# All denominators added by DMA, longer lags, and the result copied out of PSUM by VectorE

## The reference

```python
w = exp(weight_gen - max(weight_gen))          # over the 7 taps
w = w / (sum(w) + 1e-9)
x = sum_k w[b, s, h, k] * x_pad[b, s + k, h]   # 4 x 4096 tokens, 192 wide, 8 heads

h = x @ w_in                                   # 16384 x 192 @ 192 x 2048
P = a[0] + a[1] * h + a[2] * h**2 + a[3] * h**3
Q = 1.0 + abs(b[0]) * abs(h) + abs(b[1]) * h**2
out = (P / (Q + 1e-6)) @ w_out                 # 2048 x 192
```

## Time and profile before

| | |
|---|---|
| median of 3 runs | 1492.36 us (1492.22 to 1493.45) |
| profiled execution | 1492.54 us |
| its span | 1490.7 us |
| busy: PE / PEld | 1311.9 (88%) / 1175.2 (79%) us |
| busy: DVE | 1401.8 us (94%) |
| busy: ACT | 1185.8 us (80%) |
| busy: POOL | 1366.0 us (92%) |
| DMA, queue of GpSimd / of SyncE | 50.34 MB, 16.6% / 51.36 MB, 10.2% of 16 engines |
| granted TensorE clock, mean | 0.992 |

### The profile page before, as it was taken

The page is one execution under the profiler, slowest core; times in us unless marked ns, Lnnn a source line. Parts: engine busy times, 40 slices in busy tenths (PEclk is TensorE's granted clock), DMA queues, the critical chain, the costliest instruction groups (busy, mean ns, idle before and its releaser), DMA issues.

```text
span 1490.7 us, 19206 instructions
## 1 busy us (share of the span) xinstructions
PE 1311.9 (88%) x6912; PEld 1175.2 (79%) x6912; DVE 1401.8 (94%) x904; ACT 1185.8 (80%) x966; POOL 1366.0 (92%) x704
## 2 busy tenths in 40 slices
PE   0399999999999999999999999999999999998998
PEld 0278888888888888888888888888888888888897
DVE  3998999999999999999999999999999999999986
ACT  1287888888788888778788888788878888878896
POOL 1889999999999999999999999999999999999632
PEclk9899999999999999999999999999999999999999
DMA  3422322322331322331321332231232232232112
GB/s 95 124 43 65 83 69 61 82 51 66 82 80 50 82 56 61 82 82 51 79 66 51 82 82 61 69 82 43 74 82 72 58 82 53 61 79 53 29 45 64
DMA packets 26270, 101.87 MB, mean 68 GB/s; under 512 B 2968, under 2 KB 9236, under 8 KB 26256
## 3 DMA queue, kind: packets, MB, share of 16 engines
q0 software_dynamic: 9216, 50.34, 16.6%
q1 hardware_dynamic: 16752, 51.36, 10.2%
q10 hardware_dynamic: 288, 0.00, 0.0%
HBM read 38.78 MB, written 12.58 MB: 34 GB/s over the span
## 4 chain that ended last, share of the span: by engine, by line
issue 39%; POOL 31%; DMA 13%; ACT 7%; PE 5%; SPq 2%; DVE 2%; POOLq 1%; ACTq 0%
POOL prod L322 18%; DMA den<-beta 12%; POOL beta L352 6%; ACT den L451 3%; POOL conv L322 3%; PE hps L679 3%; PE ops L689 3%; ACT den L475 2%; POOL conv L326 2%; SPq L240 1%; ACT xt_hi L414 1%; POOL taps L391 1%; POOL taps L377 1%; POOL den L359 1%; DMA num<-in_moe_w_in 1%
## 5 line engine op out<-in xcount | busy, mean ns | idle before, releaser
L689 PE MATMUL ops<-wo,gate 128*128 128x192 f32 x4096 | 700.3, 327 | 49.2 <-DVE gate L604 49.2
L689 PEld LDWEIGHTS ops<-wo,gate 128*128 128x128 f32 x4096 | 673.2, 190 | 77.8 <-DVE gate L604 62.6
L326 POOL TENSOR_TENSOR conv<-conv,prod 128x768 f32<-128x768 f32 (+2 forms) x192 | 556.1, 2896 | 15.0
L604 DVE SCALAR_TENSOR_TENSOR gate<-num,coef,den 128x1536 f32<-128x1536 f32 (+1 forms) x192 | 445.7, 2321 | 4.1 <-issue 3.1
L451 ACT ACTIVATE den<-den,one_eps 128x1536 f32<-128x1536 f32 (+1 forms) x192 | 276.1, 1438 | 199.9 <-DMA den<-beta 199.0
L322 POOL TENSOR_TENSOR prod<-xwin,taps 128x768 f32<-128x768 f32 (+2 forms) x192 | 380.6, 1982 | 3.4
L623 DVE SCALAR_TENSOR_TENSOR num<-num,coef,hps 128x1536 f32<-128x1536 f32 (+1 forms) x192 | 314.3, 1637 | 6.8
L620 DVE TENSOR_TENSOR num<-num,hps 128x1536 f32<-128x1536 f32 (+1 forms) x192 | 300.4, 1565 | 13.9 <-ACT num L478 13.8
L478 ACT ACTIVATE num<-hps,coef 128x1536 f32<-128x1536 f32 (+1 forms) x192 | 285.4, 1486 | 0.0
L454 ACT ACTIVATE den<-den 128x1536 f32<-128x1536 f32 (+1 forms) x192 | 258.6, 1347 | 5.1
L352 POOL TENSOR_SCALAR beta<-den,absb 128x1536 f32<-128x1536 f32 (+1 forms) x128 | 233.5, 1824 | 30.9 <-ACT den L475 16.5
(11 more groups left out here) (53 smaller groups left out, 886.8 us busy)
## 6 DMA issues: line engine op xcount, KB each, us to landing
den<-beta POOLq DMA_DIRECT2D x64, 768.0 KB, 5.6
xwin<-in_x SPq DMA_DIRECT2D x30, 960.0 KB
out<-out_sb SPq DMA_DIRECT2D x32, 384.0 KB, 2.4
taps_raw<-in_weight_gen SPq DMA_DIRECT2D x32, 112.0 KB, 2.2
wo<-in_moe_w_out SPq DMA_DIRECT2D x1, 1536.0 KB, 13.5
num<-in_moe_w_in SPq DMA_DIRECT2D x2, 512.0 KB, 6.8
num<-in_moe_w_in SPq DMA_DIRECT2D x4, 256.0 KB, 7.7
xwin<-in_x SPq DMA_DIRECT2D x1, 768.0 KB
```

The lines of the kernel that those rows point to most:

```text
L326: pool.tensor_tensor(conv[parity][:, cols], conv[parity][:, cols], prod[k % 2][:, cols], ALU.add).then_inc(conv_steps, 1)
L604: dve.scalar_tensor_tensor(slot(gate, g), slot(num, g), coef[:, 0:1], slot(den, g), ALU.add, ALU.mult).then_inc(gate_ready, 1)
L689: last = pe.matmul(ops[:, j // 2, (j % 2) * D:(j % 2 + 1) * D], gate[:, g % GATE_RING, n * COLS + j * P:n * COLS + (j + 1) * P], wo[:, c, ...
```

## The change

All six groups are `DMA_GROUPS`, none is a `POOL_GROUP`. So ScalarE makes the scaled |h| and the square in every group, GpSimd only issues the six DMAs, and L352, L359 and L628 are gone. The lags are 2, 3 and 4 groups instead of 1, 2 and 3; `num` and `den` have four places for groups instead of three, `beta` three instead of two. For their memory the three scratch arrays of VectorE's first two convolutions share that of `gate`. The copy out of `ops` is a VectorE instruction in place of a ScalarE one, and with the longer lag it stands in g3's slot, and TensorE's wait for it in g4's. The three small instructions that make the root for the square stand earlier on VectorE, since g0 needs it.

```diff
-INVERT_LAG = 1
-GATE_LAG = 2
-LAG = 3
-RING = 3
+INVERT_LAG = 2
+GATE_LAG = 3
+LAG = 4
+RING = 4
 GATE_RING = 3
-POOL_GROUPS = (4,)
-DMA_GROUPS = (2, 5)
+BETA_RING = 3
+POOL_GROUPS = ()
+DMA_GROUPS = tuple(range(GROUPS))
...
-        beta = sb("beta", [P, 2, GW])
+        beta = sb("beta", [P, BETA_RING, GW])
         gate = sb("gate", [P, GATE_RING, GW])
+        dprod = [gate[:, n, 0:ROW] for n in range(3)]
...
@@ scalar: evacuate, and its call between the two activations of invert
-            def evacuate(s, parity, stored_needed):
-
-                act.wait_ge(gate_used, GROUPS * (s + 1))
-                if stored_needed:
-                    act.wait_ge(out_stored[parity], after_dmas(s - 2, parity))
-                act.activation(out_sb[parity][:, :].rearrange("p (c w) -> p c w", c=2),
-                               ops[:, :, 0:ROW // 2], ACT.Copy).then_inc(out_ready, 1)
...
-                            if q == EVACUATE_AT and not first:
-                                evacuate(t - 1, 1 - odd, stored_needed=not second)
...
@@ vector
+            def evacuate(s, parity, stored_needed):
+
+                dve.wait_ge(gate_used, GROUPS * (s + 1))
+                if stored_needed:
+                    dve.wait_ge(out_stored[parity], after_dmas(s - 2, parity))
+                dve.tensor_copy(out_sb[parity][:, :].rearrange("p (c w) -> p c w", c=2),
+                                ops[:, :, 0:ROW // 2]).then_inc(out_ready, 1)
...
                         dve.tensor_tensor(slot(den, g), slot(den, g), slot(beta, g), ALU.mult).then_inc(q_by_dve, 1)
+                    if q == EVACUATE_AT and not first:
+                        evacuate(t - 1, 1 - odd, stored_needed=not second)
```

More of the change, by code:

```diff
@@ L100, in conv_rational_ffn @@
         prod = [sb(f"prod{n}", [P, ROW]) for n in range(2)]
-        dprod = [sb(f"dprod{n}", [P, ROW]) for n in range(3)]
         conv = [sb(f"conv{n}", [P, ROW]) for n in range(2)]
@@ L346, in group @@
                     return
-                if not first or q >= 2:
-                    wait_q(pool, t if q >= 2 else t - 1, (q - 2) % GROUPS)
+                if not first or q >= BETA_RING:
+                    wait_q(pool, t if q >= BETA_RING else t - 1, (q - BETA_RING) % GROUPS)
                 pool.wait_ge(abs_ready, GROUPS * t + q + 1)
@@ L454, in invert, with tile @@
                 act.activation(slot(den, g), slot(den, g), ACT.Exp, scale=-1.0).then_inc(inv_q_ready, 1)
-            def tile(t, odd, first=False, second=False, xt_ahead=True, taps_ahead=True):
+            def tile(t, odd, first=False, xt_ahead=True, taps_ahead=True):
                 for q in range(GROUPS):
@@ L470, in tile @@
                         act.activation(slot(den, g), h_of(q), ACT.Abs, scale=absb[:, 0:1]).then_inc(abs_ready, 1)
-                        if not first or q >= 2:
-                            wait_q(act, t if q >= 2 else t - 1, (q - 2) % GROUPS)
+                        if not first or q >= BETA_RING:
+                            wait_q(act, t if q >= BETA_RING else t - 1, (q - BETA_RING) % GROUPS)
                         act.activation(slot(beta, g), h_of(q), ACT.Square, scale=root[:, 2:3]).then_inc(square_ready, 1)
@@ L492, in _ @@
             tile(0, 0, first=True)
-            tile(1, 1, second=True)
-            with act.Fori(2, TILES - 4, 2) as t:
-                tile(t, 0)
-                tile(t + 1, 1)
-            for t in range(TILES - 4, TILES):
+            with act.Fori(1, TILES - 3, 2) as t:
+                tile(t, 1)
+                tile(t + 1, 0)
+            for t in range(TILES - 3, TILES):
                 tile(t, t % 2, xt_ahead=t + 1 < TILES, taps_ahead=t + 3 < TILES)
@@ L500, in _ @@
                 invert(GROUPS * (TILES - 1) + q, TILES - 1, place((TILES - 1) % 2, q))
-            evacuate(TILES - 1, (TILES - 1) % 2, True)
         @block.vector
@@ L580, in _ @@
             pre_conv(0)
+            dve.wait_ge(root_guess, 1)
+            dve.reciprocal(root[:, 1:2], root[:, 0:1]).then_inc(root_inverse, 1)
+            dve.wait_ge(root_inverse, 1)
+            dve.scalar_tensor_tensor(root[:, 2:3], root[:, 1:2], absb[:, 1:2], root[:, 0:1], ALU.mult,
+                                     ALU.add).then_inc(root_twice, 1)
+            dve.wait_ge(root_twice, 1)
+            dve.tensor_scalar(root[:, 2:3], root[:, 2:3], 0.5, None, ALU.mult).then_inc(root_ready, 1)
             wi_lo_half(0)
@@ L605, in gate_of, with tile @@
                                          ALU.add, ALU.mult).then_inc(gate_ready, 1)
-            def tile(t, odd, first=False, xt_ahead=True, taps_ahead=True):
+            def tile(t, odd, first=False, second=False, xt_ahead=True, taps_ahead=True):
                 for q in range(GROUPS):
@@ L642, in _ @@
             tile(0, 0, first=True)
-            with dve.Fori(1, TILES - 3, 2) as t:
-                tile(t, 1)
-                tile(t + 1, 0)
-            for t in range(TILES - 3, TILES):
+            tile(1, 1, second=True)
+            with dve.Fori(2, TILES - 4, 2) as t:
+                tile(t, 0)
+                tile(t + 1, 1)
+            for t in range(TILES - 4, TILES):
                 tile(t, t % 2, xt_ahead=t + 1 < TILES, taps_ahead=t + 3 < TILES)
@@ L649, in _ @@
                 gate_of(GROUPS * (TILES - 1) + q, place((TILES - 1) % 2, q), True)
+            evacuate(TILES - 1, (TILES - 1) % 2, True)
         @block.tensor
```

7 lines of the change are left out of this document (removed).

## The result

| | before | after |
|---|---|---|
| median (range) | 1492.9 us (1492.22 to 1493.83) | 1601.21 us (1600.13 to 1602.62) |
| span of the profiled execution | 1490.7 us | 1598.3 us |
| tile in the settled stretch | 44.34 us | 47.78 us |
| granted TensorE clock, mean | 0.992 | 0.93 |

What follows compares the result with a forecast made beforehand. VectorE and GpSimd were taken to bound the old kernel; in the new one, 30 cycles through the late copy (1340.1 us) plus start and end gave 1511 us, and clock falls + 20: 1531 us, range 1493 to 1585.

Steps and rivals of the forecast that it cites:

- What bounded the kernel before: Settled stretch of the old kernel: VectorE and GpSimd together set the pace, at 44.34 us per tile.
- DMAs at nothing: Six DMAs per tile cost no time: landing plus a GpSimd step below 10 us, against some 14 us of cover.
- Rival (c): A DMA late, or VectorE held up by GpSimd at g3: 1540, up to 1590 with a falling clock; chance 0.08.
- ScalarE's slots, 41.05 us: ScalarE's own work over the six groups of a tile, summed to 41.05 us: the tile if nothing else came last.
- The path to the copy: From ScalarE's |h| of g3 through square, linear step and VectorE's num steps to the copy: 8.04 us, copy 0.94.
- The ring: Cycle ScalarE, VectorE's num steps, copy, TensorE's second product, back to ScalarE: 44.7 us per tile.
- rival (d): Copy ready early enough, so ScalarE's 41.05 us set the pace: 1401 us; chance 0.11 including its half, 1489.
- The end of TensorE's gap to ScalarE's |h| of g5: From TensorE's second product of g0, after waiting for the copy, to ScalarE's next three-chunk |h|: 7.68 us.
- at the edge: TensorE's new gap before the second product of g0, 4.1 us, is nearly the 4.30 us that cost the clock.
- eight of thirty: TensorE's clock falls behind the gap in eight of thirty tiles: + 20 us on 1511.
- rival (b): TensorE's clock falls behind the gap in nearly every tile: 1560 to 1590 us; chance 0.10.
- the price of a fall: Time TensorE's matmuls behind the gap lose when the clock halves: 2.5 us per tile.

## Why the prediction was wrong, step by step

- **What bounded the kernel before: held, with one reading that was too short.** VectorE and GpSimd set its pace: less of their work (copy ahead, all groups by DMA) gives 41.0 us per tile. But the 122.1 us of ScalarE for DMAs in the earlier trace rows went for another reason than the lag of two, as the runs with short lags show.
- **DMAs at nothing: right.** Three times as many, landing in 5.6 us in the median (4.4 for two chunks; 6.5 at the most from 500 to 1300 us), and no wait for one. Rival (c) did not occur.
- **ScalarE's slots, 41.05 us: right**, 41.02 where they bind. The square of two chunks, which had no row, took 1.00 (taken: 0.97).
- **The path to the copy: right**, 8.06 us (8.04), and the copy 0.95 (0.94), by the two sizes of the numerator step in the earlier trace rows.
- **The ring: right**, 44.75 (44.7) where the clock holds, and rival (d) as well in its size: with the copy out of the way 1396 where 1401 was worked out.
- **The end of TensorE's gap to ScalarE's |h| of g5: the first failed term.** 7.68 us from the earlier trace rows are those of a second product at full clock. It was 765.12 - 754.45 = 10.67.
- **The step that failed: "One gap doesn't tell how regularly such a one counts; being at the edge, I take eight of thirty".** The clock fell in all of them (0.50 behind the gap in every settled tile), and not by chance: the tile settled into a length at which each gap ends at the same distance ahead of the rise of the clock. That was rival (b), with a chance of 0.10, and its interval of 1560 to 1590 was too low as well, since the price of a fall was not 2.5 us but 3.08. The 2.5 came from the earlier trace rows, a stretch in which only 5.1 us of matmuls followed the gap, ten of them first products and four transposes; here it was a second product of 24 matmuls, slow from its first to nearly its last. 1511 + 30 x 3.08 = 1603, against 1601.21 measured.
- **Where the reasoning could have been better from the same rows.** One gap of 4.30 us was the only one of its size in the trace of before, and it took the clock; the gaps up to 2.1 us of the settled tiles never did in that trace. In some other executions of the same kernel the mean granted clock was 0.96 to 0.985 instead of 0.992, at the same 1491 to 1494 us: it fell more often there, at no cost that shows. So one trace doesn't tell how often a gap counts. A gap of 4.1 us is 0.2 from the one and 2.0 from the other. There was no row of a gap of this size that left the clock alone, and "at the edge" had no ground. What I leaned on was that equal gaps need not have equal results; that is true of 1.92 and of 3.70 us here and was not of 4.25 or 3.08. And I drew the eight of thirty as if tiles were independent of each other, though a fall shifts the next gap.
- **The Trainium skill**, page TensorE: Matmul & The Clock Gate (HAM oscillation — how this bites in real kernels): by its rule that gaps between bursts put the array at half rate, every tile would pay, 1586 in the prediction's working, and the trace agrees (0.50 behind the gap in every settled tile). That sampling which runs free of the kernel lets equal gaps come out unlike (part 1) is borne out by the run with ten more matmuls, 5.82 us in 6 tiles of 27 and 4.14 in the others, and by the one with four more copies, 5.5 to 7.2 us behind equal gaps. In the changed kernel equal gaps came out alike, since it repeats itself and settled.

## What to carry to other kernels

An instruction that another engine waits for belongs in its engine's queue at the point where its own inputs are ready, ahead of everything that waits for something later: here two positions on VectorE were worth 205 us. A standstill of TensorE that recurs in each pass is not priced by its length alone: where the trace has a gap of about that size that cost the clock, count the fall each time and price it by the matmuls that stand right behind the gap. And where an engine waits for a DMA, look first at when it was issued and what stood in front of the issue, before the distance to its use is made longer.

## What the runs showed of the hardware

- The granted clock fell to 0.50 (1.2 GHz) behind every TensorE gap of 4.25, of 3.08 and of 2.98 us in the settled tiles, behind 6 of 27 gaps of 1.92 us, and behind none of the gaps of 0.7, 0.8 or 1.5 us. With only the copy changed in the kernel before, eight of nine gaps of 3.7 us and a little more cost it, one didn't.
- The price of a fall was between 1.4 and 3.1 us for the same 24 matmuls. It went by when the gap ended and not by its length: 6.20 us behind a gap of 5.19, 7.15 behind one of 4.24, 5.62 and 7.00 in turn behind gaps of 2.98.
- A kernel whose tile contains such a gap settled on a length of 47.78 us and kept it when 0.95 us of work was added. The clock rose every 47.79 us from the first fall on, in both, while the ends of the gaps still moved. Within that reach an edit on the critical path moves the time hardly at all, so a null result there says nothing of the edit.
- Redundant matmuls in the gap gave back 89 us. As an experiment it separates the clock from the ring; as a remedy it is 116 us worse than to move the copy.
- The same instructions of VectorE and GpSimd changed their mean durations when only the result's copy was moved: L326 from 2896 to 2157 ns, the product with beta from 2477 to 2109 ns, while GpSimd's product of g4 went up from 2368 to 3760 ns (500 to 1300 us).
